# First tokens of the mixer split inside the last attention step, weight units 6 and 7 finished within the first mixer calls

## The reference

```
# stage A, per batch: linear attention, then mixing over tokens
q_s = softmax(q, over head_dim);  k_s = softmax(k, over seq)
x   = q_s @ (k_s^T @ v)                      # heads side by side: 576 x 512
u   = x + (relu(x^T @ w_tok1) @ w_tok2)^T    # w_tok1 576x256, w_tok2 256x576
# stage B, over all 4608 tokens
y   = u + relu(u @ w_ch1) @ w_ch2            # 512x1536, 1536x512
# stage C
n   = (y - mean) / sqrt(var + 1e-6) * g_ln
out = y + relu(n @ w2_ch1) @ w2_ch2          # 512x2048, 2048x512
```

## Time and profile before

| | us |
|---|---|
| three runs | 1567.18, 1562.39, 1567.74 |
| median | 1567.18 |
| profiled execution, its own time | 1563.69 |
| its span | 1561.9 |
| PE busy | 1472.2 (94% of the span) |
| VectorE busy | 1076.6 (69%) |
| ScalarE busy | 698.2 (45%) |
| GpSimd busy | 309.0 (20%) |
| one `x_hi` split on ScalarE (L566, mean) | 0.957 |
| share of PE in the chain that ended last | 74% |

### The profile page before, as it was taken

The page is one execution under the profiler, slowest core; times in us unless marked ns, Lnnn a source line. Parts: engine busy times, 40 slices in busy tenths (PEclk is TensorE's granted clock), DMA queues, the critical chain, the costliest instruction groups (busy, mean ns, idle before and its releaser), DMA issues.

```text
span 1561.9 us, 19837 instructions
## 1 busy us (share of the span) xinstructions
PE 1472.2 (94%) x7584; PEld 1322.4 (85%) x7584; DVE 1076.6 (69%) x1165; ACT 698.2 (45%) x844; POOL 309.0 (20%) x315
## 2 busy tenths in 40 slices
PE   6999896898999999899989999999999999999998
PEld 5988885787888887788878888888888888889998
DVE  7987876397486486496696687568657856872276
ACT  5656654352453453352452453344345424532342
POOL 6587785323303312300000000000000000000000
PEclk9999998899999999999999999999999999999999
DMA  7899985989989989979658767766876687667766
GB/s 241 256 306 296 299 282 202 403 318 366 354 291 379 372 294 362 352 288 317 240 184 300 248 209 266 249 247 219 275 243 228 237 277 244 211 219 256 251 214 199
DMA packets 150334, 429.28 MB, mean 275 GB/s; under 512 B 14240, under 2 KB 43488, under 8 KB 150240
## 3 DMA queue, kind: packets, MB, share of 16 engines
q1 hardware_dynamic: 132768, 361.94, 67.6%
q0 software_dynamic: 17472, 66.07, 11.8%
HBM read 348.26 MB, written 79.69 MB: 274 GB/s over the span
## 4 chain that ended last, share of the span: by engine, by line
PE 74%; DMA 10%; DVE 7%; issue 3%; SPq 2%; POOL 2%; ACT 2%; DVEq 0%; ACTq 0%; POOLq 0%
PE ps L1131 24%; PE ps L1133 23%; PE ps L1132 23%; DMA w_ring<-w_scratch_B 6%; DMA vt<-v 2%; SPq L289 2%; DMA qt<-q 1%; DVE o_lo L980 1%; DVE x_lo L834 1%; PE ps L1155 1%; DMA w_op<-w2b 1%; PE ps L1166 1%; DVE q_sum L761 1%; POOL q_lo L464 0%; DVE h L950 0%
## 5 line engine op out<-in xcount | busy, mean ns | idle before, releaser
L1131 PE MATMUL ps<-x_hi,w_ring 128*128 128x462 f32 (+1 forms) x980 | 369.2, 377 | 44.1 <-issue 15.1
L1131 PE MATMUL ps<-o_hi,w_ring 128*128 128x462 f32 (+1 forms) x980 | 367.4, 375 | 9.6 <-DVE o_lo L980 7.9
L1133 PE MATMUL ps<-x_hi,w_ring 128*128 128x462 f32 (+1 forms) x980 | 366.7, 374 | 0.0
L1132 PE MATMUL ps<-x_lo,w_ring 128*128 128x462 f32 (+1 forms) x980 | 366.7, 374 | 0.0
L1132 PE MATMUL ps<-o_lo,w_ring 128*128 128x462 f32 (+1 forms) x980 | 364.8, 372 | 0.0
L1133 PE MATMUL ps<-o_hi,w_ring 128*128 128x462 f32 (+1 forms) x980 | 364.6, 372 | 0.0
L671 ACT CAST o_hi<-h 128x924 fp32r<-128x924 f32 (+1 forms) x210 | 202.3, 963 | 254.8 <-PE ps L1133 225.0
L980 DVE TENSOR_TENSOR o_lo<-h,o_hi 128x924 fp32r<-128x924 f32 (+1 forms) x210 | 240.8, 1150 | 61.2 <-ACT o_hi L671 61.2
L1131 PEld LDWEIGHTS ps<-x_hi,w_ring 128*128 128x128 f32 x980 | 186.2, 190 | 74.3 <-issue 31.2
L1131 PEld LDWEIGHTS ps<-o_hi,w_ring 128*128 128x128 f32 x980 | 185.1, 189 | 40.1 <-issue 17.5
L950 DVE TENSOR_TENSOR h<-ps,h 128x924 f32<-128x924 f32 (+1 forms) x90 | 100.6, 1117 | 163.5 <-PE ps L1133 163.1
(11 more groups left out here) (140 smaller groups left out, 1831.3 us busy)
## 6 DMA issues: line engine op xcount, KB each, us to landing
w_ring<-w_scratch_C SPq DMA_DIRECT2D x280, 512.0 KB, 3.8
w_ring<-w_scratch_B SPq DMA_DIRECT2D x210, 512.0 KB, 5.6
w_scratch_C<-w_out POOLq DMA_DIRECT2D x8, 1792.0 KB, 11.7
w_scratch_C<-last_pair POOLq DMA_DIRECT2D x8, 1792.0 KB, 11.8
w_scratch_B<-w_out POOLq DMA_DIRECT2D x6, 1792.0 KB, 10.4
w_scratch_B<-last_pair POOLq DMA_DIRECT2D x6, 1792.0 KB, 9.9
kt<-kT SPq DMA_DIRECT2D x32, 288.0 KB, 6.0
u_scratch<-u_out SPq DMA_DIRECT2D x32, 288.0 KB, 3.8
```

What stands on the lines that cost most here:

```text
L1131: mm(dst, a_hi, b_hi, start=start, stop=False, skip_group_check=onto)
L1132: mm(dst, a_hi, b_lo, start=False, stop=False, skip_group_check=onto)
L1133: return mm(dst, a_lo, b_hi, start=False, stop=stop, skip_group_check=onto)
```

## The change

`UNITS_A` goes from 8 to 6, so units 6 and 7 are no longer finished in or behind the last step of stage A: their high halves are made behind entries 2 and 4 and their low halves on VectorE. The entries behind which units 8 to 11 are split go from 2, 5, 8, 12 to 7, 9, 12, 14; those of units 12 and up stay. GpSimd loads and sums one unit further ahead: for unit n it issues the load of unit n+2, then the store of n, then sums n+2. In `step(7, 0)` ScalarE makes all `x_hi` up to part 4, and parts 5 and 6 right behind it; VectorE makes `x_lo` 0 and 1 ahead of the low halves of r (`r_lo`, line 878), `sum_x(0, 1)` behind them, and `x_lo` 2 with `sum_x(0, 2)` behind its first copy of the output.

```diff
@@ -62,9 +62,9 @@
     ALL_ENTRIES = entries
 
 
-    UNITS_A = NB
-    HI_AT = {e: UNITS_A + i for i, e in enumerate((2, 5, 8, 12, 27, 36))}
-    HI_AT.update({(s + 1) * ENTRIES["B"] + e: UNITS_A + 6 + 5 * s + i
+    UNITS_A = NB - 2
+    HI_AT = {e: UNITS_A + i for i, e in enumerate((2, 4, 7, 9, 12, 14, 27, 36))}
+    HI_AT.update({(s + 1) * ENTRIES["B"] + e: UNITS_A + 8 + 5 * s + i
                   for s in range(3) for i, e in enumerate((0, 6, 11, 27, 36))})
     HI_AT = {e: u for e, u in HI_AT.items() if u < U0["C"] + UNITS["C"]}
 
@@ -503,19 +503,17 @@
                 sum_unit(i - 1)
                 if later:
                     lo_q(i + 1)
-                lo_unit(i - 1)
-                store_unit(i - 1)
+                    lo_unit(i - 1)
+                    store_unit(i - 1)
 
             batches(step)
-            load_unit(NB)
-            sum_unit(NB - 1)
-            lo_unit(NB - 1)
-            store_unit(NB - 1)
-            for n in range(NB, U0["C"] + UNITS["C"]):
-                sum_unit(n)
-                if n + 1 < U0["C"] + UNITS["C"]:
-                    load_unit(n + 1)
+            sum_unit(UNITS_A + 1)
+            for n in range(UNITS_A, U0["C"] + UNITS["C"]):
+                if n + 2 < U0["C"] + UNITS["C"]:
+                    load_unit(n + 2)
                 store_unit(n)
+                if n + 2 < U0["C"] + UNITS["C"]:
+                    sum_unit(n + 2)
 
 
         @block.scalar
@@ -594,6 +592,7 @@
                         exp_k(i + 1, ST[0:1])
                     else:
                         hi_x(0, 0)
+                        hi_x(0, 1)
                     hi_qT(i, ST[4:])
                     act.wait_ge(g_done, 2 * i + 2)
                     nc.scalar.copy(gT[:, 2:4, :], bank[6][:, :].rearrange("p (c n) -> p c n", c=2)).then_inc(gT_made, 1)
@@ -622,8 +621,11 @@
                             exp_k(i + 1, ST[2 + c:3 + c])
                         if c >= 1:
                             hi_q(i + 1, ST[c - 1:c])
-                    if later == 0 and c == 0:
-                        hi_x(0, 1)
+                    if later == 0 and c == 1:
+                        hi_x(0, 2)
+                        hi_x(0, 3)
+                    if later == 0 and c == 2:
+                        hi_x(0, 4)
                 if later:
                     hi_q(i + 1, ST[3:])
                 if later and not first:
@@ -690,18 +692,14 @@
                     nc.scalar.activation(ln[:, 3, 0:2 * n], ln[:, 0, 0:2 * n], ACT.Abs_reciprocal_sqrt)\
                       .then_inc(root_made, 1)
 
-            hi_unit(NB - 2)
-            for p in (2, 3):
+            for p in (5, 6):
                 hi_x(0, p)
-            hi_unit(NB - 1)
             for c in CALLS:
                 if c.j >= 0:
                     last = c.j == G1S[c.stage] - 1
                     for p in range(7):
                         if p in (0, 1, 2, 6):
                             take(c, p)
-                        if c.index == 0 and p < 3:
-                            hi_x(0, 4 + p)
                         if p == 4:
                             relu(c, 4)
                         if p == 5:
@@ -873,6 +871,10 @@
                     if later:
                         sub_k(i + 1, ST[1:3])
                         max_q(i + 1, ST[2:3])
+                if later == 0:
+                    inputs_over(dve)
+                    lo_x(0, 0)
+                    lo_x(0, 1)
                 for m in range(ND):
                     dve.wait_ge(rhi_made, ND * i + m + 1)
                     nc.vector.scalar_tensor_tensor(out=r_lo[:, m, :], in0=bank[(7, 2)[m]][:, :], scalar=0.0,
@@ -883,6 +885,8 @@
                     sub_k(1, ST[0:3])
                 elif later:
                     max_q(i + 1, ST[3:])
+                if later == 0:
+                    sum_x(0, 1)
                 for c in range(NC):
                     if later:
                         if c == 0 and not first:
@@ -905,13 +909,9 @@
                     elif later and c < 2 and not first:
                         sub_k(i + 1, ST[3 + c:4 + c])
                     if later == 0 and c == 0:
-                        inputs_over(dve)
-                        lo_x(0, 0)
+                        lo_x(0, 2)
+                        sum_x(0, 2)
                 if later == 0:
-                    lo_x(0, 1)
-                    sum_x(0, 1)
-                    lo_x(0, 2)
-                    sum_x(0, 2)
                     lo_x(0, 3)
                     lo_x(0, 4)
                     lo_x(0, 5)
```

## The result

The changed kernel takes 1577.96 us (median of five runs, 1575.62 to 1582.36) against 1566.66 us before (five runs, 1562.39 to 1567.74). The ratio is 1.0089, with a 95% interval of 1.0068 to 1.0110: slower by 0.9%, 14 us by the ratio and 11.3 by the two medians. The profiled execution is the median one, 1577.96 us round a span of 1576.2.

A forecast was written before the change was run, and what follows sets the result against it. TensorE bounds the kernel overall; at the seam PE with its holes runs almost level with the unit chain ending in unit 11's store. Entry 23's +4.2 us and the clock's 1.7 make +5.9, forecast 1573 us, range 1556 to 1585.

The forecast's parts named there:

- The holes: PE's idle before entries 2 and 5: 10.18 us shrinks to some 0.6 us, 7.82 us goes.
- the gate of unit 11's store: Entry 23's load waits for this store, which ends the chain of units; the wait was 3.7 us before.
- the main reading: The forecast at the seam: the chain of units to unit 11's store sets entry 23; 1573 us, chance 0.40.
- lo_x ahead of r_lo: VectorE in the last step: two lo_x beside GpSimd's sums make the step end 3.0 us later (0.1 to 3.4).
- Unit 6's turn: Its low half behind entries 3 and 4 ends at 262.1; only then are unit 8's load and unit 6's store issued.
- GpSimd's turns: In the seam, five turns from unit 6 to unit 11 at 11.5 us each, 57.5 us.
- Entry 23: First entry with unit 11: starts at 337.1 against 332.94, +4.2 us.
- The clock's 1.7 us: PE at the lower clock for 12 us after idling before entry 23: 1.7 us lost (0 to 3.4).
- Behind entry 23: Later stages: the new order changes no wait, costed at nothing, with 2 us either way.
- Slower turns: Rival in the seam: turns of 12.9 us and store 13.05 start entry 23 at 347.3; 1583 us; chance 0.30.
- Short turns: Rival in the seam: DMA alone the floor, entry 23 starts at 327.2; 1563 us; chance 0.20.
- holes simply gone: Rival in the seam: PE's holes go and nothing replaces them, -17.8 us; 1549 us; chance 0.10.

The follow-up runs named there:

- before_late_new: Kernel before with only the late part of the new order (load n+2, store n, sum n+2, from unit 12 on): 1575.5 us, 1.0076.
- late_old: Changed kernel with GpSimd's old order (store n, sum n+1, load n+2) from unit 12 on, the seam keeping the new one: 1567.2 us, 1.0021.
- late_adj: Changed kernel with store n, load n+2, sum n+1 from unit 12 on, the load right behind the store: 1573.8 us, 1.0053.
- gaps_ahead_again: More rounds: seam with units 6, 7 split in idle times, sum n+1 behind store n, splits at entries 6, 10, 14, 18; old order later: 1559.7 us, 0.9960.

## Why the prediction was right or wrong

The time, 1577.96, lies in the range, and the direction of the sum was right, at about half the size (+5.9 us said, 11.3 to 14 measured); but "within 0.5%" was held a little likelier (0.46) than "slower" (0.40), and slower it was. Point by point:

*The holes.* Right. Both are gone, and they were not worth their length. Entry 2 is held for 1.04 us (0.6 said). The seam does end at the gate of unit 11's store, as the main reading had it.

*lo_x ahead of r_lo.* Wrong in size, the first step that failed: "the last step ends 3.0 us later". The first entry ended 1.3 us later, of which some 0.6 is an earlier offset (GpSimd's load of unit 7 was issued at 232.83 against 232.25), so about 0.7. Counted from PE's matmuls at 233 us, the nine other profiles with this edit have 0.7 to 0.9 us (seven) and 1.6 us (two), and before_late_new, without it, has none. I had taken the row at 264.26, where GpSimd won; here VectorE had the port first, and GpSimd's first sum was the one to wait. The rule of the Trainium skill (SBUF — State Buffer, section SBUF: two separate sides), that whoever starts first keeps the pair, gave 0.5, and this trace agrees with it here: 1.33 us for GpSimd's held sum, 2.68 for the two of VectorE.

*Unit 6's turn.* The time is right, 262.1 said and 261.27 measured, but by two errors: entry 0 started 1.9 us earlier than said (244.85 for 246.7), and from there unit 6 took 16.4 us and not 15.4.

*GpSimd's turns.* Right: 11.5 us said, 11.2 measured. Store 11 was issued at 318.76 (321.0 said). PE stopped at entries 10, 13, 16 and 17 as foreseen, but for 5.31, 1.84, 1.69 and 9.72 us and not "3 to 8 us each", and at 13 it was VectorE that held it; entry 22 ended at 331.2 and not near 328.

*Entry 23.* 337.1 said, 333.15 measured, +0.2 us and not +4.2. The 4 us are five small terms: unit 6's turn 0.8 and the five turns 1.5 earlier, the issue and the landing of the store 0.8 later (10.6 us for 9.9), and the ring's load 2.5 shorter, 3.7 us for 6.3, in a stretch where DMA was at 0.71 (329.4 to 333.1) and not at 1.00 as before. The clock's 1.7 us was right: entry 23 took 4.34 us from its start to its end, 1.7 more than before (2.68). By entry 23 the sum had +5.9, and the trace +1.9. late_old, which is this part of the change alone, measures +0.2%.

*Behind entry 23.* Wrong, and this is the term that sets the result: "the new order there changes no wait that I can find, and I cost it at nothing, with 2 us either way". It costs 11 to 12 us, shown from both sides by late_old and before_late_new. I had looked only for waits on a semaphore. The order moves 512 KB to within 1.3 to 1.7 us of a 1792 KB store, fourteen times, in a stretch where DMA is at 0.93 and PE has waits of 1 to 2 us already. In the changed kernel some of these are longer (1.68 us has become 3.28 at entry 84, 1.32 has become 3.25 at entry 126), and after them the clock goes to its lower level for a time: 0.72 over 12 us round entry 84. That the load beside the store lengthens the waits is the likelier reading, not proved to be the whole, as late_adj shows; that the clock has a large part is shown by its mean over all runs, 0.985 against 0.989 to 0.990, which is 6 to 8 us. So the range held the time by luck, by two errors of opposite sign: 4 us too much in the seam and 12 too little behind it.

*The rivals.* "Slower turns" gave 1583 by turns of 12.9 us; they were 11.2, so the slower case came true by another way. "Short turns" and "holes simply gone" are out: entry 23 stayed where it was, and gaps_ahead_again shows that even with PE 15.6 us ahead the gate holds.

## What to carry to other kernels

A hole on the bounding engine is worth what the next gate leaves of it: before you cost its removal, follow each later gate (here the store of the last weight unit) back to its own start, and sum the bytes that must pass first. What PE gains ahead of the gate can still count by taking its own loads out of the way of the last store (13.05 us became 7.7). When a loop is reordered for one stage, list all stages that run it: here the order made for the 6 units of the seam was also given to the 16 behind it, and there it cost more than the seam could give. And where DMA is nearly full and the matmul engine has waits of 1 to 2 us, a wait that grows does not add its own length alone, because the clock can drop behind it. Last, count a local gain from a point just ahead of the edit: here the same code ahead of it ended up to 4 us apart in two profiles.

A version that beats both kernels, though by little, came out of this: gaps_ahead, with the splits of the tokens moved, units 6 and 7 split in idle times, and the old order from unit 12 on: 1559.7 us, 0.9960 (0.9941 to 0.9979). In its first measurement it was 0.9985 (0.9958 to 1.0011).

## What the runs showed of the hardware

VectorE against GpSimd for the port goes both ways in one program: the difference at 264.26 in the kernel before lost to sums issued 0.2 us behind it (3.33 us for one), and the two at 233.05 in the changed kernel won (2.68 us for two, first sum 1.33). In both, GpSimd was generating descriptors as VectorE came. What tells them apart stays open.

The length of a hole does not by itself tell whether the clock drops. In the changed kernel the one of 3.28 us at entry 84 did it (first matmul 0.72 us); in the kernel before the one of 3.48 us at entry 42 did not (0.45 us), and no matmul there was slow behind 304. In late_old holes of 2.55 us (at 387.13) and 1.80 us (at 639.63) did it. Nor does the first matmul tell: behind the hole of 3.25 us at 629.74 in the changed kernel it took 0.45 us, and only from 630.95 on did matmuls take 0.59 us in place of 0.37, until 634.
